# Head of an attention and two-MLP kernel: masks of two items by ScalarE copies and GpSimd selection, ends by ScalarE, one load per item with filled rows, first factors in halves, and three steps of the loop in another order

## The reference

```python
f = 1.0 / (1.0 + np.exp(-f_logit))              # (4, 8, 768, 48)
for t in range(S):                              # state: 48 x 48 for each batch and head
    state = f[:, :, t, :, None] * state + np.einsum('bhd,bhe->bhde', k[:, :, t], v[:, :, t])
    y[:, :, t] = np.einsum('bhd,bhde->bhe', q[:, :, t], state)
x = y.transpose(0, 2, 1, 3).reshape(3072, 384)
h = x @ w_in; g = where(h >= 1, h, where(h <= -1, 0, (h + 1) ** 2 / 4)); x = g @ w_out      # d_ff 2048
h = x @ w2_in; g = P(h) / (Q(h) + 1e-6); out = g @ w2_out     # P cubic, Q = 1 + |b0||h| + |b1|h^2
```

## Time and profile before

| | |
|---|---|
| median of 3 runs | 914.7 us (914.59 to 915.46) |
| the profiled execution: its own time | 913.45 us |
| its span, first to last instruction | 911.7 us |
| busy: TensorE, VectorE, ScalarE, GpSimd | 885.8, 665.3, 631.9, 271.0 us |
| mean granted TensorE clock | 0.998 |

### The profile page before, as it was taken

One profiled execution on the slowest core, in us unless ns is written; L12 is line 12 of the kernel. 1 busy time (PEld: TensorE's weight loads), 2 busy tenths in 40 slices (PEclk: granted clock), 3 DMA queues, 4 the chain that ended last, 5 costly groups with the idle time before them and its releaser, 6 DMA issues.

```text
span 911.7 us, 13158 instructions
## 1 busy us (share of the span) xinstructions
PE 885.8 (97%) x4786; PEld 732.0 (80%) x4786; DVE 665.3 (73%) x816; ACT 631.9 (69%) x822; POOL 271.0 (30%) x200
## 2 busy tenths in 40 slices
PE   4898999999999999999999999999999999999997
PEld 3787878888888888888888887888888888888886
DVE  8866666566555666565344799999899889989885
ACT  6766665655556555655567888888788888887873
POOL 3454400000100000000055385635344254343331
PEclk9999999999999999999999999999999999999999
DMA  8752122112111311200234121001001001000001
GB/s 216 192 167 59 37 68 72 36 35 87 36 36 36 98 51 35 79 26 1 84 91 137 44 63 36 1 35 35 0 35 35 12 22 35 30 5 0 35 0 38
DMA packets 26743, 48.70 MB, mean 53 GB/s; under 512 B 4544, under 2 KB 7616, under 8 KB 26688
## 3 DMA queue, kind: packets, MB, share of 16 engines
q1 hardware_dynamic: 26688, 47.99, 17.6%
HBM read 36.18 MB, written 9.44 MB: 50 GB/s over the span
## 4 chain that ended last, share of the span: by engine, by line
PE 81%; DVE 8%; ACT 4%; issue 4%; SPq 1%; DMA 1%; POOL 1%; POOLq 0%; DVEq 0%; ACTq 0%
PE acc L1233 19%; PE acc L1184 19%; PE h_pair L1167 17%; PE at_pair L1206 10%; PE h_pair L1206 10%; PE at_pair L1107 2%; PE at_pair L1126 2%; PE at_pair L1121 2%; DVE growth L869 1%; DVE g L940 1%; SPq L352 1%; DVE x_lo L933 1%; ACT t L664 1%; ACT t L661 1%; DMA q_in<-qC 1%
## 5 line engine op out<-in xcount | busy, mean ns | idle before, releaser
L559 POOL TENSOR_TENSOR g_lo<-g,g_hi 128x1024 fp32r<-128x1024 f32 x46 | 111.1, 2415 | 212.5 <-DVE t L984 212.5
L940 DVE SCALAR_TENSOR_TENSOR g<-h_pair,t 128x512 f32<-128x512 f32 x96 | 66.3, 691 | 137.0 <-ACT t L664 136.9
L661 ACT ACTIVATE t<-h_pair,half 128x512 f32<-128x512 f32 x96 | 66.0, 688 | 96.2 <-PE h_pair L1167 94.9
L1167 PE MATMUL h_pair<-x_hi,w_hi 128*128 128x512 f32 x288 | 113.0, 392 | 2.5 <-DVE x_lo L933 1.9
L522 POOL TENSOR_TENSOR k_s<-k_in,growth 128x512 f32<-128x512 f32 x22 | 28.9, 1315 | 286.0 <-DVE growth L869 268.9
L1233 PE MATMUL acc<-g_hi,w_hi 128*128 128x512 f32 x288 | 112.1, 389 | 0.3 <-POOL g_lo L559 0.3
L1167 PE MATMUL h_pair<-x_hi,w_lo 128*128 128x512 f32 x288 | 112.2, 390 | 0.0
L1167 PE MATMUL h_pair<-x_lo,w_hi 128*128 128x512 f32 x288 | 112.1, 389 | 0.0
L1233 PE MATMUL acc<-g_lo,w_hi 128*128 128x512 f32 x288 | 112.0, 389 | 0.0
L1233 PE MATMUL acc<-g_hi,w_lo 128*128 128x512 f32 x288 | 112.0, 389 | 0.0
L671 ACT CAST g_hi<-g 128x512 fp32r<-128x512 f32 x88 | 54.6, 620 | 81.5 <-DVE g L940 81.5
(11 more groups left out here) (171 smaller groups left out, 2045.7 us busy)
## 6 DMA issues: line engine op xcount, KB each, us to landing
w_raw<-w SPq DMA_DIRECT2D x32, 384.0 KB, 3.8
f_in<-fC SPq DMA_DIRECT2D x48, 96.0 KB, 2.9
k_in<-kC SPq DMA_DIRECT2D x48, 96.0 KB, 2.4
q_in<-qC SPq DMA_DIRECT2D x48, 96.0 KB, 2.3
mlp_out<-o_sb SPq DMA_DIRECT2D x18, 256.0 KB, 3.2
x_raw<-mlp_out SPq DMA_DIRECT2D x6, 768.0 KB, 4.5
outT<-o_sb SPq DMA_DIRECT2D x18, 256.0 KB, 2.0
v_in<-vC SPq DMA_DIRECT2D x22, 192.0 KB, 2.5
```

The costliest lines, as they stand in the source:

```text
L559: nc.gpsimd.tensor_tensor(g2_lo[r][:, :, :], g2[r][:, :, :], g2_hi[r][:, :, :].bitcast(F32), ALU.subtract).then_inc(lo2_ready, 1)
L661: nc.scalar.activation(t1[n % 2][:, :], h1[n % 2], ACT.Relu, scale=0.5, bias=half[:, :]).then_inc(relu1_ready, 1)
L940: nc.vector.scalar_tensor_tensor(out=g1[n % 2][:, :], in0=h1[n % 2], scalar=1.0, in1=t1[n % 2][:, :], op0=ALU.max, op1=ALU.min).then_inc(g ...
L1167: mm = nc.tensor.matmul(h1[n % 2], w[:, at:at + P], x[:, kt, cols], start=(kt == 0 and j == 0), stop=(kt == KT - 1 and j == 2))
```

## The change

1. **Masks.** For items 0 and 1 `mask` goes. ScalarE copies the scores from PSUM to `probs` (`copy_scores`, two copies for each item), and GpSimd sets what lies above the diagonal to zero in place with one selection over 1,024 columns (`select`). `outputs` waits for the selection, `transposes` for the copies. `scan(2)` and `scan(3)` stand in VectorE's list where the masks stood.
2. **Ends.** The copy to `ends` is made by ScalarE at the end of `invert`, for all 24 items.
3. **Loads.** One transfer of 128 rows for each item's f, k or q; the host fills rows 48 to 63 and 112 to 127 with copies of the head's first 16 rows. The six fills of buffers go, and with them SP's waits for them. `load_v(0)` stands behind the first four loads of f.
4. **First factors.** Item 0's exp and + 1 are made in halves of 256 columns (`first_gate`), and its scans start on the first half.
5. **Order in the head.** TensorE does `scores(2)` and `scores(3)` earlier and `deltas(0)` and `deltas(1)` later; ScalarE does `invert(3)` ahead of `round_y(0)` and `gate_steps(4)` behind the last key copies; `rest_y(0)` stands behind `mask(2)`.
6. **Order in the loop.** `newton(i + 1)` stands ahead of `spline_lo` at stage 2, where it stood behind the states; `split_w1` on ScalarE stands ahead of `spline_hi` at stages 1 to 3 and right behind it at stage 0, where it stood at the step's end.

```diff
 # SP
             def rows(dst, src, i, done):
                 chunk, r = chunk_of(i)
-                for h in range(2):
-                    sp.dma_start(dst[HS * h:HS * h + DH, :], src[r, chunk, h]).then_inc(done, 16)
+                sp.dma_start(dst[:, :], src[r, chunk]).then_inc(done, 16)
...
-            sp.wait_ge(f_pads_set, 1)
             load_f(0)
-            sp.wait_ge(f_pads_set, 2)
             load_f(1)
-            sp.wait_ge(k_pads_set, 2)
             load_k(0)
-            sp.wait_ge(q_pads_set, 2)
             load_q(0)
             load_k(1)
-            load_v(0)
             load_q(1)
             load_f(2)
             load_f(3)
+            load_v(0)
             load_v(1)
 # GpSimd
-            for u in range(2):
-                nc.gpsimd.memset(k_in[u][:, :], 0.0).then_inc(k_pads_set, 1)
...
+            def select(i):
+
+                pool.wait_ge(scores_copied, 2 * (i + 1))
+                blocks = probs[i][:, :, :].rearrange("p h (b t) -> p (h b) t", t=CK)
+                nc.gpsimd.affine_select(out=blocks, in_=blocks, compare_op=ALU.is_ge, fill=0.0,
+                                        base=0, pattern=[[0, 2 * BATCH], [1, CK]], channel_multiplier=-1).then_inc(selected, 1)
...
             scale_keys(0)
             scale_keys(1)
+            select(0)
             scale_keys(2)
+            select(1)
             scale_keys(3)
 # ScalarE
+            def first_gate():
+                act.wait_ge(f_loaded[0], 16)
+                for c in range(2):
+                    at = slice(c * NB // 2, (c + 1) * NB // 2)
+                    step = score_ps[0][c][:, at]
+                    nc.scalar.activation(step, f_in[0][:, at], ACT.Exp, scale=-1.0).then_inc(exp_done, 1)
+                    act.wait_ge(exp_done, c + 1)
+                    nc.scalar.activation(step, step, ACT.Copy, bias=1.0).then_inc(step_ready, 1)
...
+                r = chunk_of(i)[1]
+                last = growth[u][:, :].rearrange("p (b t) -> p b t", b=BATCH)[:, :, CK - 1:CK]
+                nc.scalar.copy(ends[:, BATCH * r:BATCH * (r + 1)].rearrange("p (b t) -> p b t", t=1), last).then_inc(ends_done, 1)
+
+            def copy_scores(i):
+                act.wait_ge(scores_ready, i + 1)
+                for h in range(2):
+                    nc.scalar.copy(probs[i][:, h, :], scores_at(i)[0][h]).then_inc(scores_copied, 1)
...
                 if stage == 0:
                     copy_keys(i)
+                elif n <= PIECES - HEAD_PIECES:
+                    split_w1(n + HEAD_PIECES - 1)
                 if n < N1:
                     spline_hi(n)
+                if stage == 0 and n <= PIECES - HEAD_PIECES:
+                    split_w1(n + HEAD_PIECES - 1)
                 if stage == 1:
                     invert(i + 1)
                 if stage == 2:
                     round_y(i)
                 if stage == 3:
                     gate_steps(i + 2)
-                if n <= PIECES - HEAD_PIECES:
-                    split_w1(n + HEAD_PIECES - 1)
 # VectorE
-            nc.vector.memset(f_in[0][:, :], PAD_LOGIT).then_inc(f_pads_set, 1)
-            nc.vector.memset(f_in[1][:, :], PAD_LOGIT).then_inc(f_pads_set, 1)
-            nc.vector.memset(q_in[0][:, :], 0.0).then_inc(q_pads_set, 1)
-            nc.vector.memset(q_in[1][:, :], 0.0).then_inc(q_pads_set, 1)
...
-                dve.wait_ge(growth_ready, GROUPS * (i + 1))
-                last = growth[u][:, :].rearrange("p (b t) -> p b t", b=BATCH)[:, :, CK - 1:CK]
-                nc.vector.tensor_copy(ends[:, BATCH * r:BATCH * (r + 1)].rearrange("p (b t) -> p b t", t=1),
-                                      last).then_inc(ends_done, 1)
...
-            mask(0)
             scan(2)
-            mask(1)
             scan(3)
-            rest_y(0)
             newton(2)
             scale_queries(2)
             newton(3)
             scale_queries(3)
             mask(2)
+            rest_y(0)
             mask(3)
...
                 if stage == 0:
                     mask(i)
+                if stage == 2:
+                    newton(i + 1)
                 spline_lo(n)
                 if stage == 0:
                     scan(i + 1)
@@
                     states(i)
                     if i % GROUPS == LAST:
                         rest_y(i)
-                    newton(i + 1)
                     scale_queries(i + 1)
 # TensorE
             scores(1)
             outputs(0)
             transposes(0)
+            scores(2)
             outputs(1)
+            scores(3)
             transposes(1)
-            scores(2)
+            outputs(2)
             deltas(0)
-            scores(3)
+            outputs(3)
             deltas(1)
-            outputs(2)
-            outputs(3)
             transposes(2)
```

More of the change, by code:

```diff
@@ L768, in _ @@
             nc.scalar.preload_act_table_set(ACT_TABLES)
-            gate_steps(0)
+            first_gate()
             gate_steps(1)
@@ L775, in _ @@
             gate_steps(3)
+            copy_scores(0)
             invert(2)
+            copy_scores(1)
+            invert(3)
             round_y(0)
             copy_keys(0)
-            invert(3)
             round_y(1)
             copy_keys(1)
-            gate_steps(4)
             split_w1(0)
@@ L788, in _ @@
             copy_keys(3)
+            gate_steps(4)
             split_w1(2)
@@ L1113, in outputs @@
                 y_ps = scores_at(i)[0][0]
-                pe.wait_ge(masked, 2 * (i + 1))
+                if i < 2:
+                    pe.wait_ge(selected, i + 1)
+                else:
+                    pe.wait_ge(masked, 2 * (i - 1))
                 v, loaded, count, _ = values(i)
```

32 lines of the change are left out of this document (18 added, 14 removed).

## The result

The changed kernel takes 906.5 us (median of four, 904.85 to 907.8) against 915.08 for the kernel before beside it: a ratio of 0.9907, 95% interval 0.9887 to 0.9927. That is 8.6 us less where 4.4 were forecast; the forecast time was 910.3 us, with a range from 906.7 to 913.7. The profiled execution took 904.85 us, its span is 903.1.

The account below looks back on a forecast made before the run. VectorE bounds the head, with q_in's landing just behind; waits for x_lo cost time to 120 us, then TensorE bounds. Head 1.0 plus loop 3.4 (1.35 + 1.7 + 0.35) is 4.4 us off 914.7: 910.3 us, range 906.7 to 913.7.

Parts of the forecast that it names:

- Loop, first wait: TensorE's wait for x_lo before scores near 73 us: x_lo 1.35 us earlier, wait 2.3 becomes 0.95.
- Newton 66.55 to 68.85, g_lo to 70.0, q_s 1.1: VectorE's loop chain ahead of x_lo: Newton products 1.2 and 1.1 us, q_s 1.1, contended by GpSimd's splits.
- The 0.4 us earlier g: Loop, first window: g starts 0.4 us earlier, at 65.85, 0.6 from ScalarE less 0.2 for a longer scan.
- Loop, the clock: Stretch from 75.0 to 80.3 us at mean clock 0.68: full clock comes back, saving 1.7 us.
- Loop, second and third wait: TensorE's later waits for x_lo (0.9 and 1.3 us): both stay at about 0.95, saving 0.35 us together.
- shortens by about 1.5 us a window, so the wait stays at about 0.95 and 0.95: Loop chain through one window, from cast to x_lo: about 1.5 us shorter, against a TensorE 3 us earlier.
- The bound of 6.2: Loop's upper bound: 6.2 us saved if all waits go (3.2 + 1.3 + 1.7).
- Rival B: Loads keep up and waits go: head 2.2 us, loop 5.8, time 906.7; chance 0.18.
- Head: Up to the first MLP's third product, at 35.3 instead of 36.33 us: 1.0 us saved.
- q_in of item 2: Head's loads: lands at 18.6 us, queue at 264 GB/s, two microseconds earlier with 17 SP issues instead of 28.
- Selection: GpSimd in the head: 1.7 us over 1,024 columns, between 1.1 (twice a fill) and 2.4 (eight smaller selections).
- rival C: Cold TensorE: head gives nothing or loses up to 1.8 us, loop gives 3.4; 911.3 to 913.1 us; chance 0.12.

Follow-up runs that it names:

- e1: Changed kernel with both loop-order edits taken back (Newton step behind the states, w_hi casts at the step's end): 913.3 us, ratio 0.9994 to the kernel before.
- e13: Changed kernel with unused transposes in TensorE's waits and two early w_hi casts, both loop-order edits taken back: 910.5 us, ratio 0.9945 to the kernel before.
- e5: Changed kernel with each load of f, k or q as two transfers of 64 rows: 914.3 us, ratio 1.0003 to the kernel before.
- e9: The changed kernel run once more, unaltered, on another set's chip: 906.4 us, ratio 0.9908 to the kernel before.
- e12: Changed kernel with 30 unused transposes ahead of the first scores, 18 more in later TensorE waits, first two w_hi casts early: 904.0 us, ratio 0.9883.
- e10: Changed kernel with 30 unused transposes ahead of the first scores: 906.1 us, ratio 0.9905 to the kernel before.
- e11: Changed kernel with 30 unused transposes ahead of the first scores and the first two w_hi casts early: 904.5 us, ratio 0.9888.

## Why the prediction was wrong, and where it was right

The forecast was 1.0 us for the head and 3.4 for the loop. By the two profiled executions it was 2.4 and 6.1.

**Loop, first wait: 1.35 forecast, 2.3 came.** The step that failed is the sum "Newton 66.55 to 68.85, g_lo to 70.0, q_s 1.1". It priced Newton's first product at 1.2 and q_s at 1.1, because the earlier splits would meet them; they took 0.68 and 0.69. That is 0.9 of the 1.05 us by which the chain from g to x_lo came out shorter than forecast. The 0.4 us earlier g did not come: g kept its distance to T3.

**Loop, the clock: 1.7 forecast, 1.7 came.** Right in size, and no wait, no fall. It is not a term by itself, though: in e1 and e13 the first wait (2.2 us) brings no fall, and the next wait is 2.3 us instead of 0.9, with the fall behind it.

**Loop, second and third wait: 0.35 forecast, 2.2 came.** This is the larger part of the error. The step was "shortens by about 1.5 us a window, so the wait stays at about 0.95 and 0.95". With 2.0 us less from g to x_lo in the first window alone, the chain catches TensorE there and keeps up in the next two, so nothing is left of either wait. The runs with one edit each show how steep it is: without the casts 4.4 us come back (waits of 0.8, 1.0 and 2.2 us), without the Newton step 0.9. The bound of 6.2 was in the working and came nearly true (6.1), although the wait for y_lo near 50 us grew by 0.4. Rival B had the loop at 5.8; it got 0.18.

**Head.** q_in of item 2: 18.6 forecast, 16.2 came. The step that failed is the rate: it was put at the 264 GB/s that the queue made with 48-row transfers at a share of 0.99, and with 128-row ones it made 341 and 361 at 0.98 and 1.00. That fewer issues by SP bring the load forward was right in direction (e5), but in the changed kernel the DMA engines bind, not SP. Selection: 1.7 us taken between 1.1 and 2.4, 1.09 came, so the fill was the nearer row. By the Trainium skill ("GPSIMD Engine Reference", Performance versus the Vector engine) about 1.0 had been estimated; the trace agrees with it. Score copies, exp halves and ends copies came as forecast (0.53 to 0.59, 0.37 to 0.39, 0.19). First load at 0.82 (1.0), end of q_s for item 0 at 9.66 (10.15). That q_in's landing then decides the first product was not so: it lands at 16.2 in e9 too, where that product is as late as forecast.

**Cold TensorE was rival C, and it is half true.** The 2.08 us sets were seen, and that they could cost 2 us. The forecast took the clock's course in the head as fixed by the work. It is not: of the changed kernel's executions half seem to rise by 17 us and half some five later (one profile of each group), which moves T3 by 2.3 us. In the later half the head gains 0.2 us (36.15 against 36.33), in the other 2.4; the forecast of 1.0 lies between two values that occur. That e9's first product comes at 29.46, where 29.5 was forecast, is luck: its q_in was earlier than forecast and its TensorE slower.

What stays open: why the rise comes at one time or the other after the same work up to 17.06 us, what the executions do that have no trace, and why the first Newton product and q_s were not lengthened beside a split. The head's first factors in halves and its new order were never taken back, and masks, ends and loads not on a TensorE that stays up.

## What to carry to other kernels

A chain that lags its consumer in several windows in a row should be costed to the point where it catches up: each saving beyond it removes every later wait whole, and the clock's fall behind them. Which wait the clock falls behind can change (e1), so waits and fall are better summed than priced one by one. Contention between VectorE and GpSimd is a matter of which product lies in which split; moving both moves the overlap, so it is counted product by product in a new timeline, not carried over at the old row's price. Where TensorE starts from rest, look at a second execution before reading the head's times, and try unused products in its waits: e12, with these and two casts moved, has a median 2.4 us below that of the changed kernel beside it.

## What the runs showed of the hardware

- A load of 64 rows of 2 KB takes SP 0.60 us to issue, one of 128 rows 0.43, one of 48 rows 0.45: two halves cost nearly three times the whole.
- With the DMA engines' share at 0.99 the queue moved 264 GB/s where f, k and q came in transfers of 48 rows (before, 10 to 20 us), and at 1.00 361 GB/s where they came in transfers of 128 (changed, 10 to 15 us).
- After the same TensorE work, one execution was at the higher clock level by 17.1 us and another not until after 21.0 (sets of 16 products of 1.16 and 2.08 us). The granted clock read 1.00 ahead of the first rise in both.
- A wait of 2.2 us near 72 us brought no fall of the clock in e1, one of 2.3 near 74 did in the kernel before (0.68 from 75.0 to 80.3).
- With 30 unused transposes ahead, TensorE was at the higher level by 9.8 us and fell behind a wait of 1.9 us (e10; 2.0 in e11); with 18 more in its waits it stayed up to the end of the head, through waits of 1.28 and 1.31 us (e12, one profiled execution each).
